# Attention pairs: queries and keys of both heads turned and split together, then spread by transfers inside SBUF

## The reference

```
q, k, v: (4 batches, 8 heads, 576 rows, 64)        float32
scores = q @ k.T / sqrt(64)
keep scores >= rowmax - tau, the others to -1e9
attn   = exp(scores - rowmax); attn /= sum + 1e-9
out    = attn @ v                                   -> x (2304 tokens, 512)
# mixture: x routed by argmax of normalised x @ emb.T to one of 8 experts
# y = gate * relu(x @ w1[e]) @ w2[e]
# dense:  (prelu(y @ w_in) with alpha) @ w_out
```

## Time and profile before

| | |
|---|---|
| median of 3 runs | 1100.82 us (1100.55 to 1101.2) |
| the profiled execution's own time | 1100.25 us |
| its span, first to last instruction | 1098.5 us |
| TensorE's mean granted clock, as a share of full | 0.977 |
| busy over the span | PE 93%, DVE 53%, ACT 39%, POOL 32% |
| the attention's stretch | up to about 390 us |

### The profile page before, as it was taken

How to read it: one execution, slowest core, us unless ns; L and a number is a source line. 1 busy time by engine, 2 the same in 40 slices (tenths; PEclk the granted TensorE clock), 3 DMA queues, 4 the chain that set the end, 5 groups by cost and what they waited for, 6 DMA issues and landing times.

```text
span 1098.5 us, 19741 instructions
## 1 busy us (share of the span) xinstructions
PE 1023.5 (93%) x6661; PEld 900.2 (82%) x6662; DVE 577.3 (53%) x1333; ACT 431.0 (39%) x844; POOL 347.1 (32%) x459
## 2 busy tenths in 40 slices
PE   3999999999999939999999998999999999999995
PEld 2888888888888828888888886999999999999994
DVE  4888888888888831122121223754444444444441
ACT  3777777777777602322222222322111121211111
POOL 2133324312111259899975555001010010100101
PEclk8999999999999959999999999999999999999998
DMA  6433343434320145655644436200100001000000
GB/s 174 99 68 88 88 113 98 106 93 109 88 63 20 53 150 172 205 180 193 203 152 143 174 94 204 83 20 29 29 24 26 10 29 29 29 0 0 29 1 29
DMA packets 131256, 96.00 MB, mean 87 GB/s; under 512 B 106540, under 2 KB 106572, under 8 KB 130676
## 3 DMA queue, kind: packets, MB, share of 16 engines
q1 hardware_dynamic: 116660, 66.17, 21.6%
q0 software_dynamic: 5168, 17.10, 4.4%
q10 hardware_dynamic: 9360, 11.83, 3.3%
HBM read 76.69 MB, written 17.90 MB: 86 GB/s over the span
## 4 chain that ended last, share of the span: by engine, by line
PE 70%; DVE 4%; ACT 2%; issue 2%; DMA 1%; SPq 0%; POOL 0%; ACTq 0%; DVEq 0%
PE bank L619 64%; PE bank L622 6%; ACT exps L926 1%; DVE neg_max L1138 1%; DVE probs L1149 0%; ACT probsT L964 0%; ACT q_st L946 0%; DMA x_row<-x_sorted 0%; DMA part_logit<-x_tail_sb 0%; DVE q_st L1167 0%; DVE kl_st L1177 0%; POOL out L610 0%; DVE q_st L1175 0%; SPq L403 0%; DVE X L1193 0%
## 5 line engine op out<-in xcount | busy, mean ns | idle before, releaser
L619 PE MATMUL bank<-x_hi,ring 128*128 128x384 f32 x768 | 212.2, 340 | 3.2 <-DVE x_lo L1427 3.2
L619 PE MATMUL bank<-ring,g_hi 128*128 128x512 f32 x576 | 177.5, 389 | 0.0
L1082 ACT ACTIVATE g_hi<-act 128x384 fp32r<-128x384 f32 x96 | 50.4, 525 | 301.3 <-DVE act L1486 301.3
L506 POOL TENSOR_TENSOR ring<-stage,ring 128x2048 fp32r<-128x2048 f32 x32 | 147.3, 4604 | 4.8 <-POOL ring L504 0.2
L619 PEld LDWEIGHTS bank<-x_hi,ring 128*128 128x128 f32 x768 | 140.9, 189 | 6.1 <-issue 3.4
L1483 DVE TENSOR_SCALAR neg<-bank,alpha_col 128x384 f32<-128x384 f32 x96 | 59.3, 618 | 143.0 <-PE bank L619 143.0
L619 PE MATMUL bank<-x_lo,ring 128*128 128x384 f32 x384 | 129.6, 338 | 0.0
L1149 DVE SCALAR_TENSOR_TENSOR probs<-bank,thresh,exps 128x576 f32<-128x576 f32 x144 | 117.1, 815 | 20.0 <-ACT exps L926 9.2
L619 PEld LDWEIGHTS bank<-ring,g_hi 128*128 128x128 f32 x576 | 106.9, 188 | 15.9
L1138 DVE TENSOR_REDUCE neg_max<-bank 128x1 f32<-128x576 f32 x144 | 108.2, 752 | 20.4 <-PE bank L619 18.7
L619 PE MATMUL bank<-probsT,vraw 128*64 128x128 f32 (+1 forms) x1440 | 105.5, 277 | 13.0 <-DVE X L1193 6.1
(11 more groups left out here) (184 smaller groups left out, 1634.1 us busy)
## 6 DMA issues: line engine op xcount, KB each, us to landing
stage<-in_moe_w SPq DMA_DIRECT2D x32, 1024.0 KB, 5.5
qraw<-in_q SPq DMA_DIRECT2D x64, 128.0 KB, 2.9
kraw<-in_k SPq DMA_DIRECT2D x64, 128.0 KB, 3.1
x_row<-x_sorted ACTq DMA_DIRECT2D x23, 264.0 KB, 3.9
y_sorted<-y_row ACTq DMA_DIRECT2D x21, 256.5 KB, 3.5
y_got<-y_sorted POOLq DMA_DIRECT2D x18, 256.0 KB, 3.0
vraw<-in_v SPq DMA_DIRECT2D x32, 128.0 KB, 2.6
stage<-in_moe_w_in SPq DMA_DIRECT2D x4, 1024.0 KB, 5.1
```

The costliest lines, as they stand in the source:

```text
L506: nc.gpsimd.tensor_tensor(lo, src, hi.bitcast(F32), ALU.subtract).then_inc(piece_lo, 2)
L619: return nc.tensor.matmul(dst, lhsT, rhs, start=start, stop=stop)
L1082: nc.scalar.activation(g_hi[f % 3][:, :], act2[f % 2][:, :], ACT.Copy).then_inc(g_hi_ready, 1)
```

## The change

- q and k are loaded once. Both heads stand side by side in 128 columns, so that one turn yields head 0 in partitions 0 to 63 and head 1 in 64 to 127. A pair has three groups: q (four turns), k (four turns), tails (two turns). ACT writes `q_hi` or `k_hi`, DVE `q_lo` or `k_lo`, each buffer existing once.
- New in SP's list: `spread`, 24 transfers from SBUF to SBUF per pair that place and double these parts in `q_st`, `kh_st` and `kl_st` (4 for group 0, 8 for group 1, 12 for group 2), each counted in `dup_in`. Scores of a pair wait for all 24.
- `group_of` now says: group 0 of pair n+2 in unit 3, group 1 in unit 4, group 2 of pair n+1 in unit 0. In pair 0, pair 1's groups are turned in units 0 to 2 instead of ahead of the loop.
- The probabilities of both heads stand in one row of 1152; head 1's keys are put in with its tail first, so the last 64 keys of both heads are neighbours and are turned at once into the values bank. v gets one tail chunk for each arrangement. The tail unit's second head needs its keys in two pieces (224 and 64 columns).
- The turned output goes into the free columns of a score bank. PE waits for the second mask of the unit before it.
- ACT: both exponentials come first, and `split` comes behind `copy_a`. DVE: it waits for head 1's scores before `normalise`; logits and output are normalised in one operation of 144 columns. Rows of X hold the logits between the outputs and grow from 528 to 592 numbers; a tail is stored by two transfers, not four.

```diff
-GROUPS_PREP = 5
+GROUPS_PREP = 3
+TURNED = P + 2 * EXPERTS
+XL = HEADS // 2 * TURNED
+XC = XL + 16
+Q_LOADS, V_LOADS, DUPS = 16 * 3, 16 * 5, 16 * 24
+TURN_AT = 2 * SEQ // MAIN
...
-            m, g = (n + 1, j + UNITS - FIRST_PREP) if j < FIRST_PREP else (n + 2, j - FIRST_PREP)
+            if n == 0 and j < GROUPS_PREP:
+                return 1, j
+            m, g = {MAIN - 1: (n + 2, 0), MAIN: (n + 2, 1), 0: (n + 1, 2)}.get(j, (PAIRS, 0))
...
+            def spread(n, par, g):
+
+                sp.wait_ge(split_lo, GROUPS_PREP * n + g + 1)
+                if n >= 2:
+                    sp.wait_ge(scores_ready, TILES_PAIR * (n - 1))
+                q_main, k_main = slice(0, MAIN * P), (slice(0, MAIN * P), slice(TAIL, SEQ))
+                q_tail = (slice(MAIN * P, SEQ), slice(SEQ, WIDE))
+                k_tail = (slice(MAIN * P, SEQ), slice(0, TAIL))
+                own = slice(0, MAIN * P) if g < 2 else slice(MAIN * P, SEQ)
+                for x in range(2):
+                    head = slice(x * HEAD, (x + 1) * HEAD)
+                    for half in range(2):
+                        rows = slice(half * HEAD, (half + 1) * HEAD)
+                        if g != 1:
+                            sp.dma_start(q_st[par][rows, x, q_tail[x] if g else q_main].bitcast(F32),
+                                         (q_hi, q_lo)[half][head, own].bitcast(F32)).then_inc(dup_in[par], 16)
+                        if g:
+                            to = k_tail[x] if g == 2 else k_main[x]
+                            sp.dma_start(kh_st[par][rows, x, to].bitcast(F32), k_hi[head, own].bitcast(F32)).then_inc(dup_in[par], 16)
+                            sp.dma_start(kl_st[par][rows, x, to].bitcast(F32), k_lo[head, own].bitcast(F32)).then_inc(dup_in[par], 16)
...
             load_qk(1, 1)
+            for g in range(GROUPS_PREP):
+                spread(0, 0, g)
             load_pieces(sp, 0, 0)
...
             def body(n, par):
+                if n:
+                    for m, g in ((n + 1, 1), (n + 1, 2)):
+                        if m < PAIRS:
+                            spread(m, m % 2, g)
+                else:
+                    for g in range(GROUPS_PREP):
+                        spread(1, 1, g)
                 if n + 2 < PAIRS:
                     sp.wait_ge(qk_turned, GROUPS_PREP * n + GROUPS_PREP)
                     load_qk(n + 2, par)
...
                     store_tail(n - 1)
+                if n + 2 < PAIRS:
+                    spread(n + 2, par, 0)
...
                 if j == 0 and h == 0:
-                    pe.wait_ge(split_lo, GROUPS_PREP * (n + 1))
+                    pe.wait_ge(dup_in[par], DUPS * (half + 1))
...
             def turn_last_keys(n, j):
...
+                turn(bank[:, M_BANK, P:2 * P], probs[:, MAIN * P:WIDE]).then_inc(probs_turned, 1)
...
                     turn_probs(n, j, 0)
+                    if j < MAIN:
+                        pe.wait_ge(probs_ready, tile_no(n, j, 1) + 1)
                     if not (static(n) and j < 2):
                         turn_out(*((n, j - 2) if j >= 2 else (n - 1, j + UNITS - 2)))
...
+                    values_before(n, par, half, j)
                     job = group_of(n, j)
                     if job:
                         m, g = job
+                        pe.wait_ge(split_lo, GROUPS_PREP * m + g)
+                        prep(m, m % 2, m // 2, g)
```

More of the change, by code:

```diff
@@ L232, in build @@
         split_hi = sem("split_hi")
+        dup_in = [sem(f"dup_in{i}") for i in range(2)]
         split_lo = sem("split_lo")
@@ L384, in load_qk @@
                 for raw, view, done in ((qraw[par], q_p[n], q_in[par]), (kraw[par], k_p[n], k_in[par])):
[L385 to L388, removed]
+                    sp.dma_start(raw[0:TAIL, MAIN, :, :], view[:, MAIN * P:SEQ, :].rearrange("h r d -> r h d")).then_inc(done, 16)
             def load_v(n, par):
@@ L691, in values @@
                 pe.wait_ge(probsT_ready, turn_no(n, j, 2) + 1)
[L692 to L694 removed]
+                if not (static(n) and j == 0):
+                    pe.wait_ge(outT_ready, UNITS * n + j)
+                tail = probsT[buf][:, 2 * MAIN * P:2 * SEQ]
                 if j < MAIN:
@@ L721, in turn_out @@
                 pe.wait_ge(outT_ready, UNITS * n + j + 1)
+                if not (static(n) and j == 0):
+                    pe.wait_ge(x_ready, UNITS * n + j)
                 for g in range(3):
@@ L773, in _ @@
             scores(0, 0, 0, 0, 1)
-            for g in range(UNITS - FIRST_PREP):
-                prep(1, 1, 0, g, FIRST_BANKS[g])
             pe.wait_ge(route_const, 7)
@@ L992, in _ @@
                 split(0, 0, g, FIRST_BANKS[g])
-            for g in range(UNITS - FIRST_PREP):
-                split(1, 1, g, FIRST_BANKS[g])
             for n in range(PAIRS):
@@ L1276, in pair @@
                 for j in range(UNITS):
-                    job = None if static(n) and j < 2 else group_of(*before(*before(n, j)))
-                    if job and j == MAIN:
-                        split(job[0], 1 - par, job[1])
-                    for h in heads_of(j):
-                        maxima(n, j, h)
-                        if h == 0 and job and j < MAIN:
-                            split(job[0], 1 - par, job[1])
-                        if h == 0 and not (static(n) and j < 3):
-                            for g in range(3):
-                                if (n, j) == route_unit(g, 8):
-                                    route_step(g, 7)
-                            normalise(*((n, j - 3) if j >= 3 else (n - 1, j + UNITS - 3)))
+                    job = None if static(n) and j < UNITS else group_of(*before(*before(n, j)))
+                    maxima(n, j, 0)
+                    if job:
+                        split(job[0], job[0] % 2, job[1])
+                    if j < MAIN:
+                        dve.wait_ge(scores_ready, tile_no(n, j, 1) + 1)
+                    for g in range(3):
+                        if (n, j) == route_unit(g, 8):
+                            route_step(g, 7)
+                    if not (static(n) and j < 3):
+                        normalise(*((n, j - 3) if j >= 3 else (n - 1, j + UNITS - 3)))
+                    if j < MAIN:
+                        maxima(n, j, 1)
                     for h in heads_of(j):
@@ L1293, in pair @@
                         inverse(*before(n, j))
+                    if n == 0 and 1 <= j <= GROUPS_PREP:
+                        split(1, 1, j - 1)
                     for g in range(3):
```

266 lines of the change are left out of this document (117 added, 149 removed).

## The result

The changed kernel takes 1207.88 us (1205.12 to 1208.45, 4 runs); the kernel before took 1100.97 us beside it (1100.55 to 1101.2, 4 runs). The ratio is 1.0967, with a 95% interval of 1.0948 to 1.0986. The forecast was 1180 us with a range of 1133 to 1205: the direction and the way were right, the size was not, and the median lies 2.9 us above the range. The profiled execution took 1207.61 us, its span is 1205.9 us, TensorE's mean granted clock 0.949 (0.977 before).

A forecast was written before the change was run, and what follows sets the result against it. TensorE came first before the change, VectorE not far behind; afterwards a chain through SP's loads and spreads was to bound each pair. 1100.25 + 19.8 (start) + 60.3 (loop) + 1.1 - 1.3 (end) = 1180.2, forecast 1180 us, range 1133 to 1205.

The forecast's parts named there:

- What bounds the loop: From SP's loads of one pair to the next: load, landing, splits and spreads in one chain, 27.3 us per pair.
- the signs named ahead: SP without gaps over 3 us, 37 issues per pair, TensorE idle 3 to 4 us before q, VectorE under 75%.
- The start: Up to pair 2's first turn: first mask ends near 34.5 us, q there at 65.8 instead of 46.03; cost +19.8 us.
- Part 3: The loop between successive pairs' loads on SP: 5.1 + 22.2 = 27.3 us against 22.66, +60.3 over 13 intervals.
- rival A: TensorE's clock falls in every wait for q, slowing work behind it: 28.6 us per pair, 1197 us; chance 0.25.
- the sign named for rival A: A granted TensorE clock of 0.8 or less in the attention.
- The end and behind: From pair 15's turns to the last mask 43.4 us, +1.1; last rows stored by two transfers, -1.3; later stages 0.
- TensorE's savings: 14 turns fewer per pair, 1.7 us each pair, 27 us in 16 pairs; entered as 0 because TensorE waits elsewhere.
- the turned output's wait: On TensorE, turned output waiting for the second mask: at most 10 us if TensorE bounded, entered as 0.
- the 435 GB/s: Skill page's rate between SBUF and SBUF, by which a pair's 1.67 MB of spreads would take 3.8 us, hidden.

The follow-up runs named there:

- the loads first: Changed kernel with the loads of q and k for pair n+2 at the head of a pair's body, ahead of the 20 spreads: 1170.22 us.
- four transfers more: Changed kernel with four more 2 KB transfers into a scrap buffer behind the 12 spreads of each pair's tails: 1248.91 us.
- v elsewhere: Changed kernel with the five transfers of v per pair issued by GpSimd instead of SP: 1205.31 us.
- warm turns: Changed kernel with 24 idle turns of the identity on TensorE ahead of each wait for q from pair 2 on: 1196.01 us.
- the loads first and the keys joined: Changed kernel with loads at the head of the body and one transfer spreading k's high and low parts, 16 spreads per pair: 1120.51 us.

## Why the prediction was right in kind and short in size

- **What bounds the loop: right.** The chain loads, landing, split of q, split of k, spreads, next loads was there in each of the 13 rounds, TensorE stood in unit 3 for q, and SP's issue of a spread took 0.597. The runs with the loads first, with four transfers more and with v elsewhere each move the way the chain says, though the first gave 28 us less than expected. Of the signs named ahead, 37 issues per pair and VectorE under 75% (61% in the loop) came; SP's longest gap was 3.2 us where 3 was named.
- **The start: right to 1.3 us.** The first mask ended at 34.1 (34.5 forecast), the first turn of pair 2 came at 67.08 (65.8).
- **The loop: 60.3 forecast, 81.3 measured.** This is the term that failed, the sum of 27.3 us per pair in "Part 3". Its chain was right, but it priced every round at full clock and every issue undisturbed. Measured as means of the 13 rounds:
  - From the loads to TensorE's turns of q 5.64 (5.05 to 7.61) instead of 5.1, since some issues of the loads are held: +7.0 us in all.
  - From the turns to the end of VectorE's split of q 4.88 instead of 4.1, since the turns take 1.09 and not 0.65 and the score steps 0.24: +10.1.
  - From there to the end of the split of k 4.84 instead of 5.25: -5.3. This piece was priced too long.
  - From there to the next loads 13.55 instead of 12.85, the 20 spreads and what is held among them: +9.1.
- **What the clock and the held issues have in it.** The warm turns brought the end of the split of k from 9.72 to 8.73 behind the turns of q, and the loop back by 10.5 us. In the one round of the changed kernel whose turns ran at full pace (the last rows of this document) it came at 8.82. The held issues are the first and the last of the four pieces, about 16 us: between 67.08 and 442.93, 21 of SP's 483 issues took over 0.75 us, together 15.6 us more than 0.60 each. So the held issues cost no less than the clock, and no term of the prediction had them, though the longest issue of a load in its own row was 2.078. The two are more than the 21 us that were missing, because a full-clock round was priced 0.6 us too long up to the split of k.
- **The clock: weighed the wrong way.** Rival A had this part of the mechanism and, at 28.6 per pair and 1197 us, nearly the size, but only a chance of 0.25. What spoke against it, a clock of 1.00 over 16.4 us of standing in pieces, said nothing of one piece of 4 to 6 us. After's clock over the loop is 0.90; the sign named for rival A, 0.8 or less, was set too low for a clock that is at half in only a part of each round. By the Trainium skill's rule ("TensorE: Matmul & The Clock Gate", section "HAM oscillation — how this bites in real kernels"), a wait for a DMA in every round sends the clock back each time; the trace agrees, with the turns of q at the half clock in 12 of the 13 rounds. A rule that describes the very shape of the loop forecast should have had the larger chance. The time itself lay 11 us above rival A's too.
- **The end and behind: 5 us short.** From pair 15's turns to the last mask's end it took 45.8 (43.4 forecast), in part the same slow work behind the wait. Behind the mask it took 718.9 (1207.61 - 488.73) against 717.3 before, where 1.3 less was forecast. Executions of one kernel differ by up to 3 us, so this last part can't be told from nothing, and its cause stays open.
- **TensorE's savings: rightly entered as 0 here, but real.** The change holds a gain that its first part buries: without the new q and k it is 15.6 us faster than the kernel before beside it. The prediction looked at the turned output's wait only as a cost (up to 10 us) and never at the wait it removes.
- **A slip without effect.** The spreads of a pair move 1.77 MB (12 of 128 KB and 12 of 16 KB), not 1.67; only the sentence on the 435 GB/s used it.
- **The range** reached to rival A plus 8 us. Clock and held issues are separate and add up. With rival A's 17 and only the 7 us held in the loads, 1180 is already 1204, so a range up to 1205 left no room above a case that had a chance of one in four.

## What to carry to other kernels

When a transfer moves behind others in a queue, write the round as one chain, from its issue back to its issue, and price every transfer by the queue's time per issue (0.64 us here), whatever its size, plus something for held issues (1.2 to 3.2 us per pair here); then take issues out by joining patterns before looking at bytes. A wait of 4 to 6 us in every round cost TensorE its full clock here as well, so the work behind such a wait is to be priced at half speed, above all if it stands in the chain. And a change of several parts is to be tried part by part: here the new way of q and k cost 122 us, some 20 of them by the place of one split, and hid 15 that the other parts gained.

## What the runs showed of the hardware

- SP's issue of a transfer inside SBUF takes 0.60 us for 2 KB, 16 KB and 128 KB alike (medians of 597 ns). Single issues are held and take longer, up to 2.5 us (1.98, 1.42, 1.05 in the rows above): 21 of 483 over 0.75 us in the changed kernel, and 59 of 390 with the loads first and the keys joined. Some come in a long run of issues, others as the third one behind a pause. What holds them wasn't tried apart: too many transfers under way is a guess.
- In one of the 13 rounds the clock was still full behind the wait and fell after it. TensorE's timeline in the changed kernel: 4.08 us of standing, turns and scores at full pace for one microsecond, and then the half clock (four turns in 0.96 instead of 0.60).

```profile
299.65 0.63 PE L648 MATMUL bank<-ident,qraw 128*128 128x128 f32 x4 [4.08 <-DMA qraw<-in_q]
...
300.52 0.30 PE L645 MATMUL bank<-kl_st,q_st 128*128 128x288 f32 x1
300.65 0.96 PE L648 MATMUL bank<-ident,probs 128*128 128x128 f32 x4
301.40 0.68 PE L645 MATMUL bank<-turner,outT 128*128 128x144 f32 x2
```

- Turns of the identity, which compute nothing, kept the clock up here: 24 of them ahead of each wait brought the mean clock from 0.949 back to 0.975, that of the kernel before being 0.977. In the loop the turns of q ran at full pace in 12 of the 13 rounds.
